# The third stage's weights laid 16 bytes apart, and the fourth stage moved behind the third in each half

## The reference, cut to what matters

```python
S, D = 12480, 128                       # tokens, channels
h = relu(pos_emb @ w1) @ w2 * exp(-0.01 * pos)      # a filter as long as the sequence
u = x * v
y = irfft(rfft(u, 2*S) * rfft(h, 2*S))[:S]          # causal convolution, per channel
z = x * y
g = relu(z @ moe_w_in) ** 2;   z1 = g @ moe_w_out    # 128 -> 2048 -> 128
q = z1 @ moe2_w_in;  out = (q * sigmoid(1.702 * q)) @ moe2_w_out
```

## Time and profile before

| | us |
|---|---|
| median of 3 runs | 1504.84 (1504.59 to 1507.27) |
| the profiled execution | 1502.83 |
| its span | 1501.0 |
| PE busy | 1477.3 (98%) |
| ACT / DVE / POOL busy | 999.2 / 914.5 / 197.3 |

### The profile page before, as it was taken

The page is one execution under the profiler, slowest core; times in us unless marked ns, Lnnn a source line. Parts: engine busy times, 40 slices in busy tenths (PEclk is TensorE's granted clock), DMA queues, the critical chain, the costliest instruction groups (busy, mean ns, idle before and its releaser), DMA issues.

```text
span 1501.0 us, 22451 instructions
## 1 busy us (share of the span) xinstructions
PE 1477.3 (98%) x7970; PEld 1434.4 (96%) x7970; DVE 914.5 (61%) x1198; ACT 999.2 (67%) x1404; POOL 197.3 (13%) x192
## 2 busy tenths in 40 slices
PE   8999999999999999999999999999999999999998
PEld 6987998899989999999999999999999999999997
DVE  3668576663556666666666666666666566666664
ACT  6643254323577777777777777777777777777775
POOL 5418802602300000000000000000000000000000
PEclk9999999999999999999999999999999999999999
DMA  8223503405100000000000000000000000000000
GB/s 224 74 78 110 154 1 93 124 1 158 46 1 12 12 11 11 11 11 11 11 11 11 11 12 19 15 11 11 11 11 11 11 11 11 12 11 11 6 6 12
DMA packets 28344, 52.06 MB, mean 35 GB/s; under 512 B 3060, under 2 KB 22140, under 8 KB 28052
## 3 DMA queue, kind: packets, MB, share of 16 engines
q1 hardware_dynamic: 27768, 51.02, 11.5%
q10 hardware_dynamic: 540, 0.55, 0.1%
HBM read 45.17 MB, written 6.39 MB: 34 GB/s over the span
## 4 chain that ended last, share of the span: by engine, by line
PE 96%; DVE 1%; DMA 1%; ACT 1%; issue 1%; SPq 0%; ACTq 0%
PE ps L1008 24%; PE ps L1010 24%; PE ps L1009 24%; PE ps L751 6%; PE ps L741 6%; PE ps L786 5%; PE ps L408 3%; PE ps L722 2%; DMA f_ring<-in_fwd 1%; PE ps L715 1%; DVE act_lo L996 1%; PE ps L707 0%; PE ps L729 0%; ACT act_f L951 0%; DVE act_hi L994 0%
## 5 line engine op out<-in xcount | busy, mean ns | idle before, releaser
L996 DVE TENSOR_TENSOR act_lo<-act_f,act_hi 128x832 fp32r<-128x832 f32 x480 | 489.1, 1029 | 126.8 <-ACT act_hi L954 118.5
L1008 PE MATMUL ps<-in_hi,w_hi 128*128 128x416 f32 x960 | 338.4, 353 | 6.4 <-DVE in_lo L968 2.6
L1008 PE MATMUL ps<-act_hi,w_hi 128*128 128x416 f32 x960 | 339.0, 353 | 0.9 <-DVE act_lo L996 0.9
L1009 PE MATMUL ps<-act_lo,w_hi 128*128 128x416 f32 x960 | 337.5, 352 | 0.0
L1010 PE MATMUL ps<-act_hi,w_lo 128*128 128x416 f32 x960 | 336.7, 351 | 0.0
L1010 PE MATMUL ps<-in_hi,w_lo 128*128 128x416 f32 x960 | 336.3, 350 | 0.0
L1009 PE MATMUL ps<-in_lo,w_hi 128*128 128x416 f32 x960 | 336.2, 350 | 0.0
L994 DVE CAST act_hi<-act_f 128x832 fp32r<-128x832 f32 x240 | 143.7, 599 | 296.9 <-ACT act_f L949 296.9
L944 ACT ACTIVATE relu<-ps 128x832 f32<-128x832 f32 x240 | 208.3, 868 | 131.7 <-PE ps L1010 127.4
L951 ACT ACTIVATE act_f<-ps 128x832 f32<-128x832 f32 x240 | 207.0, 862 | 107.5 <-PE ps L1010 107.3
L949 ACT ACTIVATE act_f<-relu 128x832 f32<-128x832 f32 x240 | 215.9, 900 | 22.1 <-DVE act_lo L996 0.4
(11 more groups left out here) (79 smaller groups left out, 1118.9 us busy)
## 6 DMA issues: line engine op xcount, KB each, us to landing
f_ring<-in_fwd SPq DMA_DIRECT2D x52, 240.0 KB, 2.6
big<-in_x_by_channel SPq DMA_DIRECT2D x16, 390.0 KB
big<-in_v_by_channel SPq DMA_DIRECT2D x16, 390.0 KB
out<-yT SPq DMA_DIRECT2D x30, 208.0 KB, 1.9
t<-in_inv SPq DMA_DIRECT2D x15, 338.0 KB
big<-in_pos_emb SPq DMA_DIRECT2D x40, 78.0 KB
x_tile<-in_x_by_tile SPq DMA_DIRECT2D x15, 208.0 KB, 2.6
t<-in_x_by_tile SPq DMA_DIRECT2D x15, 208.0 KB, 2.5
```

What stands on the lines that cost most here:

```text
L996: nc.vector.tensor_tensor(lo[:, :, :], f[:, :, :], hi[:, :, :].bitcast(F32), ALU.subtract)\
L1008: nc.tensor.matmul(to, w_hi[w][:, cols], hi, start=first, stop=False)
L1009: nc.tensor.matmul(to, w_hi[w][:, cols], lo, start=False, stop=False)
```

## The change

What it does, part by part:

- **P** gets a place of its own, not ZU's, and the layout [group of 4 channels, re/im, frequency, 4 channels]: a channel's 104 frequencies lie 16 bytes apart. `combine_p` writes it in runs of 16 bytes. P, Z, Y, U, the kept results X and the MLPs' weights are laid out anew in one buffer.
- **Stage 3's** DVE pair walks its elements in another order, the channel innermost, so that it writes runs of four channels.
- **Stage 4** runs behind the third stage of each half, for that half's channels alone: 15 groups in the first half, 10 in the second, 8 products each (before, 12 units of 16), with one PSUM bank and one ACT copy for a group (`keep_xy`) to X[h]. Five groups instead of three units are left for the MLPs' first tile, at positions 2, 4, 6, 16 and 17, copied by DVE. `y_made` and its spare products now come in both halves.
- **SP**: the second round of `f_ring` is loaded ahead of the other DMAs. In the first half, the first four tables `t4` and then all eight pieces of x and v are issued behind stage 2; tables 4 to 14 come after the last piece. Two of the four `t4` slots of the first half lie in `f_ring`, so `f_ring` is refilled for the second half only behind the fourth stage. Weights 0 to 2 are loaded at once behind the second stage of the second half.
- **POOL** starts U of the second half only when P is made.
- **The MLPs' input**: the two halves of a tile's rows lie in X[0] and X[1] at other partitions, so each tile costs two more DMAs of 64 rows, from X to `xy_tile`, and POOL multiplies `xy_tile` with `x_tile`.

```diff
-LATE = 3
-EARLY = [*range(JG - LATE), JG]
-LATE_AT = {2: JG - 3, 4: JG - 2, 6: JG - 1}
+LATE = 5
+LATE_AT = {2: JG - 5, 4: JG - 4, 6: JG - 3, 16: JG - 2, 17: JG - 1}
 TAB = 2 * A
...
-U_SLACK = 3 * 2 * FG * 2 * HC
+Z_SIZE = A * 2 * HC
+Y_SIZE = LOW * 2 * D
+X_SIZE = LOW * A
+XV = 2 * PC * B
+SPEC = 3 * 2 * FG * 2 * HC
...
+H_AT = BIG - D * BR
+Z_AT = (0, Z_SIZE), (Z_SIZE, H_AT + HC * BR - Z_SIZE)
+P_AT = 2 * Z_SIZE, 0
+Y_AT = 2 * Z_SIZE - Y_SIZE, 2 * Z_SIZE + X_SIZE
+X_AT = 2 * Z_SIZE, 0
+U_AT = 2 * Z_SIZE, 0
...
+IM_AT = HC * BR, SPEC_AT[1] + SPEC + RING * TB * TAB + TAB
+T4_AT = SPEC_AT[1] + SPEC
+XV_AT = ([Z_SIZE + i * XV for i in range(6)] + [U_AT[0] + HC * BR + i * XV for i in range(2)],
...
-    P = [carve(big, B, (h + 1) * Y_HALF, A, 2, HC)[0] for h in range(2)]
-    Y = [carve(big, A, h * Y_HALF, LOW, 2, 2, HC)[0] for h in range(2)]
...
+    P = [carve(big, B, at, HC // 4, 2, A, 4)[0] for at in P_AT]
+    Y = [carve(big, A, at, LOW, 2, 2, HC)[0] for at in Y_AT]
+    H, _ = carve(big, A, H_AT, D, BR)
+    U = [carve(big, A, at, HC, BR)[0] for at in U_AT]
...
         rows = ds(k * FG, FG)
-        s, x = prod_s[h][:, half], prod_x[h][:, half]
-        tensor_tensor(P[h][:, rows, 0, :], s[:, :, 0, :], s[:, :, 1, :], ALU.subtract)
-        tensor_tensor(P[h][:, rows, 1, :], x[:, :, 0, :], x[:, :, 1, :], ALU.add).then_inc(p_done[half], 1)
+        to = P[h][:, :, :, rows, :].rearrange("p g r f c -> p r f g c")
+        s, x = (prod[h][:, half].rearrange("p f r (g c) -> p r f g c", c=4) for prod in (prod_s, prod_x))
+        tensor_tensor(to[:, 0], s[:, 0], s[:, 1], ALU.subtract)
+        tensor_tensor(to[:, 1], x[:, 0], x[:, 1], ALU.add).then_inc(p_done[half], 1)
...
+    def step4(pe, h, g, q, done):
+
+        pe.wait_ge(t4_in[g % RING], 16 * (h * T4_USES[g % RING] + g // RING + 1))
+        blocks = [(0, i, t4[h][g % RING][:, i]) for i in range(TB)]
+        if g == JG - 1:
+            pe.wait_ge(t4_last_in, 16 * (h + 1))
+            blocks.append((1, TB - 1, t4_last[h]))
+        for bank, i, table in blocks:
+            to = ps[:, 2 * q + bank, i * A:(i + 1) * A]
+            for r in range(2):
+                mm = nc.tensor.matmul(to, Y[h][:, TB * g + i, r].rearrange("p m c -> p (m c)"),
+                                      table[:, r * A:(r + 1) * A], start=r == 0, stop=r == 1)
+        mm.then_inc(done, 1)
+
+    def keep_xy(copy, h, g, q):
+
+        to, made, last = X[h][:, g], ps[:, 2 * q, 0:TN], ps[:, 2 * q + 1, TN - A:TN]
+        if g < JG - 1:
+            return copy(to, made)
+        low, high = slice(h * HC, (h + 1) * HC), slice((1 - h) * HC, (2 - h) * HC)
+        copy(to[:, 0:TN - A], made[:, 0:TN - A])
+        copy(to[low, TN - A:TN], made[low, TN - A:TN])
+        return copy(to[high, TN - A:TN], last[high])
...
+    def load_xy(sp, t):
+
+        n, g = t % 2, t // 2
+        sp.dma_start(mlp["x_tile"][n][:, :], x_t[:, t * TN:(t + 1) * TN]).then_inc(x_t_in[n], 16)
+        for h in range(2):
+            rows = slice((t + h) % 2 * HC, ((t + h) % 2 + 1) * HC)
+            sp.dma_start(mlp["xy_tile"][n][h * HC:(h + 1) * HC, :], X[h][rows, g]).then_inc(x_t_in[n], 16)
...
+        def load_t4_behind(h, groups):
+
+            for g in groups:
+                s = g % RING
+                sp.wait_ge(full[s], used["s4", h][s] + g // RING)
+                load_t4(sp, h, g)
...
         for h in range(2):
-            if h == 0:
-
-                stage_done(sp, "s1", 0)
-                load_u(1, 0)
-                load_u(1, 1)
-            else:
+            for s in range(RING):
+                load_f(h, 1, s)
+            if h == 1:
 
...
+            with sp.Fori(2, F_FULL) as i:
                 for s in range(RING):
                     load_f(h, i, s)
...
             p_made(sp, h)
             stage_done(sp, "s2", h)
             if h == 0:
+                for g in range(RING):
+                    load_t4(sp, 0, g)
+                for i in range(PIECES):
+                    if i >= X_SLOTS:
+
+                        sp.wait_ge(u_folded, PIECES + i - X_SLOTS + 1)
+                    load_u(1, i)
+                    if i == X_SLOTS - 1:
+                        sp.dma_start(t4_last[0], inv4[:, JG * TB * TAB:]).then_inc(t4_last_in, 16)
+                load_t4_behind(0, range(RING, JG))
+
+                stage_done(sp, "s4", 0)
                 for s in range(RING):
                     sp.dma_start(f_ring[:, s], fwd2_d[:, s * FG:(s + 1) * FG, :]).then_inc(ld_f[s], 16)
-                load_u(1, 2)
-                for i in range(X_SLOTS, PIECES):
-
-                    sp.wait_ge(u_folded, PIECES + i - X_SLOTS + 1)
-                    load_u(1, i)
-        load_w(0)
-        sp.dma_start(mlp["x_tile"][0][:, :], x_t[:, 0:TN]).then_inc(x_t_in[0], 16)
-        y_made(sp, 1)
-        load_w(1)
-        for g in range(RING, JG):
-            sp.wait_ge(s4_full, s4_units(g - RING))
-            load_t4(g)
-            if g == RING + 3:
-
-                load_w(2)
-            if g == RING + 5:
-                load_w(3)
+        for m in range(3):
+            load_w(m)
+        stage_done(sp, "s3", 1)
+        load_w(3)
+        load_t4_behind(1, range(RING, RING + 2))
+
+        s4_done(sp, 0)
+        sp.wait_ge(free[0], used["s4", 1][0] + 1)
+        load_xy(sp, 0)
+        load_t4_behind(1, range(RING + 2, JG - 1))
 
     @block.gpsimd
     def _(pool):
...
             if h == 0:
+
+                p_made(pool, 0)
+                stage_done(pool, "s2", 0)
+                nc.gpsimd.memset(U[1][:, :, LOW:ODD], 0.0)
                 for i in range(PIECES):
                     make_u(1, i)
         for part in range(SPLITS):
             split_low(0, part)
-        pool.wait_ge(xt_low, 1)
-        pool.wait_ge(x_t_in[0], 16)
-        nc.gpsimd.tensor_tensor(mlp["stage"][:, :], XT[:, 0], mlp["x_tile"][0][:, :], ALU.mult).then_inc(staged, 1)
+        pool.wait_ge(x_t_in[0], 3 * 16)
+        nc.gpsimd.tensor_tensor(mlp["stage"][:, :], mlp["xy_tile"][0][:, :], mlp["x_tile"][0][:, :], ALU.mult)\
+            .then_inc(staged, 1)
...
-        make_hi(0)
-        for g in range(JG - LATE):
-            act.wait_ge(s4_full, g + 1)
-            copy_low(g, g % RING)
...
+            for g in range(JG - h * LATE):
+                q = g % RING
+                if h == 1 and g in HI_AT:
+                    make_hi(HI_AT[g])
+                if h == 1 and g == FIRST_HI_AT:
+                    act.wait_ge(staged, 1)
+                    nc.scalar.copy(mlp["in_hi"][0][:, :], mlp["stage"][:, :]).then_inc(x1_hi, 1)
+                act.wait_ge(full[q], used["s4", h][q] + g // RING + 1)
+                keep_xy(nc.scalar.copy, h, g, q).then_inc(free[q], 1)
...
-                low, high = (Y[h][:, 0:LOW - 1, :, m, c4].rearrange("p j r c -> p c r j") for m in (h, 1 - h))
-                re2 = re.rearrange("p c (r j) -> p c r j", r=2)[:, :, :, 1:LOW]
-                im2 = im_copy[h][:, k % 2].rearrange("p c (r j) -> p c r j", r=2)[:, :, :, 0:LOW - 1]
+                low, high = (Y[h][:, 0:LOW - 1, :, m, c4].rearrange("p j r c -> p r j c") for m in (h, 1 - h))
+                re2 = re.rearrange("p c (r j) -> p r j c", r=2)[:, :, 1:LOW, :]
+                im2 = im_copy[h][:, k % 2].rearrange("p c (r j) -> p r j c", r=2)[:, :, 0:LOW - 1, :]
...
-                    mm = nc.tensor.matmul(slot[q][0:A, e // 2, at:at + W3], P[h][:, :, r, 4 * k + e],
+                    mm = nc.tensor.matmul(slot[q][0:A, e // 2, at:at + W3], P[h][:, k, r, :, e],
                                           t3[:, r * (LOW + 1):r * (LOW + 1) + W3], start=True, stop=True)
...
+            for k, spare in ((N3 - 4, 1), (N3 - 3, 2), (N3 - 2, 2)):
+                q = k % RING
+                pe.wait_ge(free[q], used["s3", h][q] + k // RING + 1)
+                spare_products(q, spare)
+            y_made(pe, h)
+            for g in range(JG - h * LATE):
+                q = g % RING
+                pe.wait_ge(free[q], used["s4", h][q] + g // RING)
+                step4(pe, h, g, q, full[q])
+
+    def late_step4(pe, g, q):
+
+        step4(pe, 1, g, q, s4_late)
+
+    def late_keep(g, q):
+
+        keep_xy(nc.vector.tensor_copy, 1, g, q).then_inc(late_copied, 1)
...
-            sp.dma_start(x_tile[t % 2][:, :], x_t[:, t * TN:(t + 1) * TN]).then_inc(x_t_in[t % 2], 16)
-
-        sp.wait_ge(s4_full, s4_units(JG - LATE - 1))
-        load_x(1)
+        for q in range(RING):
+            banks_free(sp, q)
+        load_xy(sp, 1)
```

More of the change, by code:

```diff
@@ L163, in conv_buffers, with raw_weights @@
     }
+def raw_weights(sb):
+    w_raw, end = [None] * 4, 0
+    for m, at in ((3, X_SIZE + DFF), (0, Z_AT[1][0]), (1, Z_AT[1][0] + 2 * DFF), (2, Z_AT[1][0] + 4 * DFF + 3 * TN)):
+        sb(f"below_w_raw{m}", at - end)
+        w_raw[m] = sb(f"w_raw{m}", DFF)[:, :]
+        end = at + DFF
+    return w_raw
 def mlp_buffers(sb, F32R):
@@ L180, in mlp_buffers @@
```

(55 more changed lines are left out.)

210 lines of the change are left out of this document (71 added, 139 removed).

## The result

| | before | after |
|---|---|---|
| median of 18 runs each, us | 1504.56 | 1511.31 |
| the profiled execution, us | 1502.83 | 1511.55 |
| its span, us | 1501.0 | 1509.8 |
| third stage, one PE instruction, us | 0.180 | 0.192 |

The ratio after to before is 1.0064, with a 95% interval of 1.0046 to 1.0083: slower by 0.6%, where 1465 was forecast.

The account below looks back on a forecast made before the run. PE was taken to bound the kernel, its third stage by strided weight loads. The terms -39.2 - 2.75 - 1.8 + 1.8 + 5 - 2.5 = -39.45 gave 1463.4 profiled, 1465 us as median; range 1455 to 1490.

Parts of the forecast that it names:

- The stride, -39.2: Third stage, both halves: weights 16 instead of 512 bytes apart cut 512 instructions from 0.180 to 0.104 us, 39.2 us less.
- The lower bound, 0.104: Third stage: the pitch in us per PE instruction if the columns set the pace; the forecast took this value.
- The upper bound: Third stage: a pitch of 0.180 us, as before, so the stride would gain 0 at worst.
- The first rival: Third stage: the stride gives nothing, as any weight not beside the last costs double; -4.25 us in all, 1500.6; chance 0.15.
- `f_ring` in the second half, 0: Second half: PE's 1.56 us wait for a refill left as it is; it may go, or grow by as much.
- The MLPs' start, -2.5: First MLP tile: PE's waits of 1.0 us for ACT and 1.5 us for in_lo go; 2.5 us less (0 to 4).
- The barrier, +1.8: Between third and fourth stage: it comes twice at 2.3 us, DVE's pair shorter by 0.5, instead of once at 2.8.
- The end of the second stage and `f_ring` in the first half, -4.55: First half: POOL starting U later saves 2.75 us of PE's idle time, the earlier `f_ring` round 1.8 us.
- POOL's combine, 0: Second stage: POOL writing runs of four channels stays hidden behind PE; no cost taken, at a factor 1.4 12 us.
- the rival of a slower POOL: Second stage: POOL's combine becomes the bound, at twice today's work 53 us more, 1518; chance 0.04.
- The wait for table 4, +5: First half's fourth stage: PE waits about 4 us for table 4, plus 1 for the clock; absent with a slow third stage.
- Its 1 us for the clock: First half: a lower granted clock after the table wait could cost up to 1.5 us; 1 was taken.

Follow-up runs that it names:

- e1: The changed kernel with third-stage weights read at 18 distances, 1 to 128 floats; pitch 0.104 us at 1 float, 0.103 at 2, 0.141 at 3, 0.191 at 4.
- e4: The changed kernel with the second half's five fourth-stage table loads issued behind the last `f_ring` load; 1504.38 us, ratio 1.0016.
- e7: e4 with POOL making the low parts of the second weight ahead of the first MLP tile's input; 1499.01 us, ratio 0.9970.
- e5: e2 with e4's table order, DVE's old element order, 9 spare products ahead of the fourth stage instead of 5, and e7's edit; 1480.73 us, ratio 0.9847.
- e2: The changed kernel with P in runs of two channels, its weights 8 bytes apart; 1509.96 us, ratio 1.0043.
- e12: e5 with four first-half tables issued for each of the last two pieces, `x_tile` loaded early and one more second-half table ahead; 1472.20 us, ratio 0.9790.
- e9: e5 with one first-half table issued ahead of the seventh piece, three ahead of the last, and one more second-half table ahead; 1481.23 us, ratio 0.9837.
- e6: e2 with e4's table order and 15 spare products ahead of the fourth stage in place of 5; 1491.30 us, ratio 0.9916.
- e3: The changed kernel with P in its own place but in before's layout, weights 512 bytes apart; ratio 1.0016, three executions at 1502.9 to 1504.5 us.
- e10: The kernel before with 2, 3 and 4 spare products ahead of its fourth stage instead of 1, 2 and 2; 1502.7 to 1506.3 us, ratio 1.0004.

## Why the prediction was wrong, point by point

- **The stride, -39.2: this step failed.** The lower bound, 0.104, was right as to what is to be had, but not at this distance. The choice between the bounds went by nearness on a straight scale, "four elements apart is nearer to the side by side rows than to 128 apart". e1 shows a step, not a slope: 0.103 at 8 bytes, 0.191 at 16. Measured, the term is +6.35 (+3.03 and +3.32). The upper bound failed as well: 16 bytes costs 288 ns where 512 cost 273, so "at worst 0" was not the worst. (The product itself is 39.0 with its own pitches, not 39.2.) The point that the text itself names, "wrong above all if the pitch is not 0.104", is the one.
- **The first rival had the outcome of this term, not its mechanism nor the time.** "Any weight that isn't beside the last one" fails at 8 bytes, which are free; the rule of 16-byte lines, named beside it, holds. Its sum was -4.25 in the terms of the profiled execution, and the span moved by +8.8, 13.0 above it. Of that 6.35 is the dearer distance, 3.9 the wait for `f_ring`, 1.1 the waits for tables, 0.4 the barriers and 5.0 the MLPs' start; the tiles behind it give back 4.0. These 4.0 are in no term of the prediction: that after is only 0.6% above before is in part luck.
- **`f_ring` in the second half, 0: mis-sized.** "It may go, or grow by as much" had the direction, but it grew by more: 3.83 us against 1.56, +2.3, with 1.6 of low clock behind it. e4 shows the queue as its cause.
- **The MLPs' start, -2.5: wrong in its sign, +2.5.** The wait for ACT (1.01) went and the waits inside the first tiles fell from 6.1 to 4.4, but DVE's late copy stands behind units slowed by POOL: PE waits 3.59 for it and then runs 12 instructions at the lower clock, so that the start takes 3.5 us more with the 1.3 of moved products counted. e7 has 5 us of this back. The earlier trace rows had the same slowing, 2.18 us against 0.42, and it was used for one join alone.
- **The barrier, +1.8: 3.2.** DVE's pair did not get shorter by 0.5; each of its operations takes 0.90 us, start to start, not 0.58. The first stage's copy has one operand and the pair's operations have two: the earlier trace rows compared unlike operations, and the old 0.82 was the nearer row.
- **The end of the second stage and `f_ring` in the first half, -4.55: right**, -4.65 measured; DVE's last combine took 0.42 us and the wait before the third stage is 0.46.
- **POOL's combine, 0: right.** 728 ns each, as before, so the rival of a slower POOL has nothing for it, and the runs of 16 bytes cost DVE and POOL nothing there.
- **The wait for table 4, +5.** With the slow third stage it was said to be absent, and is (0.57). With the fast one e5 has it, 5.75 us at just that table, which PE could use 7.1 us behind the issue of the last piece, against 6.4 worked out. Its 1 us for the clock was far off: with the wait, the stage takes 24.1 us longer than after's, 18.3 of them by the clock. Even had the pitch been 0.104, the forecast would have been missed: e2 is the change with a fast stride, and took 1510.

## What to carry to other kernels

Lay what PE loads as weights 4 or 8 bytes apart, and measure a price between two rows instead of interpolating it; a hardware price by distance can be a step. Before a stage is made faster, look at what stands at its end: here waits of 1 to 6 us (a lagging DVE, a table behind pieces in SP's queue) cost little themselves, and up to 25 us by the clock in the fourth stage behind them. A term "off the path" is to be checked against every row in which the same two engines meet.

## What the runs showed of the hardware that was not expected

- **In no trace here did the fourth stage get its clock back.** 104 columns behind 128 weights, PE busy without a gap, ran at 0.50 for 52 us in e2, while the first stage's 208 columns were at 1.00 within 5 us. Waits of 0.2 to 0.8 us in that stage left the clock alone; 1.2 to 1.3 left it in one place and lost it in others (1.21 kept it in e12's second half; 1.18, 1.20 and 1.27 lost it in e9's second, in e12's first and in e6's second); the three of 2.2 us and more, in e9, e6 and e5, lost it. At the barrier 1.43 to 1.57 kept it in after and in e4, and 1.45 and 1.44 lost it in e3 and e7. What separates the cases in the middle is open.
- **Before's rare 1543 us executions** are probably the same, though this is inferred, with e3's profile at 0.970 as the nearest picture: e10, which only fills the join, had none in ten, and the size fits. At the lower clock 32 instructions take 6.83 us instead of 3.58, which for before's 392 instructions is an estimate of 40 us; these executions lie 39 above the others.
- **Some distances are dearer than the flat 272 ns**: 287 at 4 floats, 290 at 8, 292 at 9, 321 at 12, 289 at 20, 304 at 24, 284 at 127. Why these was not tested, and all but the first rest on one group of 16 instructions.
- **DVE beside POOL**: an operation on two operands in SBUF slows threefold (1.02 to 3.09 us), a cast two and a half times (0.58 to 1.43).
